# Attention with decay: a full reciprocal instead of a backward scan, the products moved to VectorE, four input buffers, one pass for transposing and gating

## The chip, the cores and the metric

The kernel runs on one core of one Trainium2 chip. The metric is the device time in microseconds, as the median of several runs. The engines are called here as the profile calls them: PE (TensorE), PEld (its weight loads), DVE (VectorE), ACT (ScalarE), POOL (GpSimd) and SP (SyncE, which issues the DMAs).

## The reference, cut to what matters

Three layers follow each other. The change touches the first alone.

```python
# q, k, v, alpha: (B, H, S, D) = (4, 8, 768, 48), fp32; alpha in 0.8 .. 1.0
state = np.zeros((B, H, D, D))
for t in range(S):
    state = alpha[:, :, t, :, None] * state + np.einsum('bhd,bhe->bhde', k[:, :, t], v[:, :, t])
    y[:, :, t] = np.einsum('bhd,bhde->bhe', q[:, :, t], state)
x = y.transpose(0, 2, 1, 3).reshape(B * S, H * D)          # (3072, 384)
logits = x @ w_gate                                        # (3072, 8)
# every token goes to one of 8 experts, best logits first, 384 tokens an expert;
# expert: relu(x @ w1[e]) @ w2[e];  after it: (silu(x @ w_gate2) * (x @ w_val)) @ w_out
```

## The kernel before, in words

**Units.** The attention cuts the 768 tokens of each batch into CH = 6 chunks of P = 128. A unit is one chunk of one batch; there are UNITS = 24, in the order chunk by chunk, and within a chunk batch by batch. `unit(i, j)` gives its number u = 4i + j, its batch b and its chunk c. The 8 heads of 48 channels lie as PAIRS = 4 pairs: the even head of a pair on partitions 0 to 47, the odd one on 64 to 111. The tokens lie along the free dimension, so q, k and alpha of a unit are each 128 x 512 values.

**The algebra.** Within a chunk, `decay` is the running product of alpha from the chunk's start (a scan along the tokens, L197, which starts each pair anew with the constant DECAY_UNIT). q is multiplied by it (`q_dec`, L261) and k by its inverse (`k_und`, L263). The inverse is not taken element by element: L204 takes the reciprocal of the last product of each pair alone (4 values a partition), and a second scan (L206) multiplies it by alpha backward from the chunk's end. For that the tokens of k, v and the scores' rows lie in reversed order, and a second, reversed copy of alpha is loaded. `qka_in` therefore holds 2052 words a row: q, k, alpha with a starting word for each pair, and alpha reversed.

**The rest of a unit.** PE multiplies `k_und` by `q_dec` (L359, `front`), which gives the scores, and turns `k_und` into rows of tokens (L366). DVE masks the scores (L215). PE's `outputs` adds two products in `ps_y_cols`: the state of the chunks before by `q_dec` (L376) and v by the masked scores (L383). For L376 ACT first writes the state of both heads of a pair into the two diagonal blocks of `state_pair` (L303), so that one product serves two heads. PE's `update` makes the chunk's share of the state (L393); DVE's `advance` adds it (L225) and scales the state with the chunk's decay (L229). ACT copies `ps_y_cols` to `y_cols` (L296). PE's `gate_and_turn` multiplies `y_cols` by the gate's weights (L401, 8 columns) and transposes it (L404). ACT copies the rows (L314, two copies) and the logits (L320), and SP stores the rows to `x_rows`.

**The order of work.** Each engine has its own stream of instructions, run in order and held by waits on semaphores. DVE's step j masks unit j+1 (`mask_scores`), makes the decays of unit j+3 (`decays`) and advances the state of unit j. PE's step j does `outputs(j)`, `update(j)`, `gate_and_turn(j-1)` and `front(j+2)`. POOL's `scale` follows the decays. SP loads unit u+2 when the keys of unit u have been scaled (`load_next`), since there are two `qka_in` buffers, then the next v of the batch, and then stores unit j. PE begins with WARMUPS = 22 matmuls on zeros.

**Beside the attention** run parts of the later layers: in each chunk two pieces of weights of 128 x 1152 are loaded and split into a high and a low part; the high parts are made by ACT (L1186), the low parts by DVE and POOL, one each (`split_gated_low`, L1190). The names `quick_...` from L631 on belong to the routing. It starts when the attention's block has ended on all engines, and its first instruction (L650) reads the finished `logits`. It and the expert layers stand behind the attention in time.

## Time and profile before

| | us |
|---|---|
| median of 3 runs | 970.67 |
| lowest and highest run | 968.34, 971.88 |
| the profiled execution, its own time | 969.62 |
| its span, from the first to the last instruction | 967.8 |
| first scan of the attention starts | 8.22 |
| first instruction of the routing starts | 204.66 |

All times inside the kernel come from the one profiled execution, counted from the start of its span. Its own time is 1.8 us longer than its span. The mean granted clock of PE over the span is 0.931 of full speed. Busy times of one engine do not add to those of another, as the engines run side by side; what a change is worth is read from the waits in its stretch.

### The profile page before, as it was taken

How to read it: one execution, taken by the hardware profiler on the slowest of the kernel's cores; microseconds unless marked ns; L12 is line 12 of the kernel's file. 1: busy time of each engine (PE TensorE's matmuls, PEld its weight loads, DVE VectorE, ACT ScalarE, POOL GpSimd, SP SyncE). 2: the span in 40 equal slices, each digit the busy share in tenths (PEclk: the TensorE clock that was granted, in tenths of full speed). 3: DMA queues.
4: the chain of work that ended last, by engine and by line, in shares of the span. 5: the costliest groups of instructions: out<-in, count | busy, mean ns of one | idle time of the engine just before them, and what ended most of it. 6: DMA issues, size and time to landing. Idle time of an engine off the chain costs nothing.

```text
span 967.8 us, 17835 instructions
## 1 busy us (share of the span) xinstructions
PE 880.0 (91%) x6586; PEld 836.5 (86%) x6586; DVE 547.3 (57%) x1077; ACT 299.2 (31%) x579; POOL 269.2 (28%) x195
## 2 busy tenths in 40 slices
PE   6798889841999999999999999999999999999991
PEld 3787878830999999999999999999999999999991
DVE  4988888846456446544644564465446445642330
ACT  1243343421323323333224233323332242333220
POOL 2444434411304140521224041305212240513001
PEclk7697798765899999999999999999999999999996
DMA  9787898604003101200220040013002200400000
GB/s 226 141 193 162 194 217 199 145 26 155 1 1 123 42 16 65 90 24 0 81 73 24 0 130 33 16 65 89 24 0 81 73 24 0 135 33 11 1 1 28
DMA packets 25250, 71.30 MB, mean 74 GB/s; under 512 B 4288, under 2 KB 10816, under 8 KB 22848
## 3 DMA queue, kind: packets, MB, share of 16 engines
q1 hardware_dynamic: 22144, 61.42, 24.9%
q0 software_dynamic: 3072, 9.44, 2.9%
q8 instruction: 20, 0.33, 0.2%
q14 instruction: 14, 0.11, 0.0%
HBM read 61.41 MB, written 9.44 MB: 73 GB/s over the span
## 4 chain that ended last, share of the span: by engine, by line
PE 72%; DVE 3%; issue 1%; DMA 1%; POOL 0%; ACT 0%; POOLq 0%; DVEq 0%; ACTq 0%
PE ps_up L1500 43%; PE ps_acc L1500 25%; PE ps_turn L784 2%; DVE quick_marks_space L709 1%; DMA x_tok<-x_rows,from_rows 1%; PE ps_turn L804 1%; PE ps_turn L1506 0%; PE ps_turn L789 0%; DVE quick_marks_space L761 0%; POOL out L1348 0%; PE ps_up L1506 0%; PE ps_acc L1506 0%; POOL x_tok L1320 0%; DVE quick_cut L708 0%; DVE quick_base L703 0%
## 5 line engine op out<-in xcount | busy, mean ns | idle before, releaser
L1326 POOL TENSOR_TENSOR w_low<-w_raw,w_high 128x768 fp32r<-128x768 f32 x60 | 134.3, 2244 | 295.9 <-ACT w_high L1390 295.4
L1500 PE MATMUL ps_up<-z_high,gated_high 128*128 128x384 f32 x576 | 198.0, 344 | 0.2 <-DVE z_low L1457 0.2
L1500 PE MATMUL ps_up<-z_high,gated_low 128*128 128x384 f32 x576 | 193.5, 336 | 0.0
L1500 PE MATMUL ps_up<-z_low,gated_high 128*128 128x384 f32 x576 | 193.3, 336 | 0.0
L1500 PEld LDWEIGHTS ps_up<-z_high,gated_high 128*128 128x128 f32 x576 | 108.2, 188 | 0.9 <-ACT z_high L1403 0.5
L1500 PEld LDWEIGHTS ps_up<-z_high,gated_low 128*128 128x128 f32 x576 | 108.3, 188 | 0.0
L1500 PEld LDWEIGHTS ps_up<-z_low,gated_high 128*128 128x128 f32 x576 | 108.1, 188 | 0.0
L1462 DVE TENSOR_TENSOR act_out<-ps_up,act_out 128x384 f32<-128x384 f32 x96 | 53.5, 558 | 94.6 <-ACT act_out L1406 91.9
L1409 ACT CAST u_high<-act_out 128x384 fp32r<-128x384 f32 x96 | 49.3, 514 | 160.3 <-DVE act_out L1466 160.3
L1500 PE MATMUL ps_acc<-gated_high,u_high 128*128 128x384 f32 x288 | 97.6, 339 | 0.3 <-DVE u_low L1469 0.3
L1500 PE MATMUL ps_acc<-gated_low,u_high 128*128 128x384 f32 x288 | 97.2, 337 | 0.0
L1500 PE MATMUL ps_acc<-gated_high,u_low 128*128 128x384 f32 x288 | 97.0, 337 | 0.0
L1406 ACT ACTIVATE act_out<-ps_up 128x384 f32<-128x384 f32 x96 | 47.3, 492 | 154.7 <-PE ps_up L1500 154.7
L1348 POOL DMA_INDIRECT out<-o_tok,to_rows x24 | 23.6, 985 | 224.7 <-ACT o_tok L1418 189.8
L1469 DVE TENSOR_TENSOR u_low<-act_out,u_high 128x384 fp32r<-128x384 f32 x96 | 53.6, 558 | 55.7 <-ACT u_high L1409 55.7
L1451 DVE SCALAR_TENSOR_TENSOR h_low<-ps_up,h_high 128x384 fp32r<-128x384 f32 x64 | 35.7, 557 | 83.3 <-ACT h_high L1386 81.2
L1466 DVE TENSOR_TENSOR act_out<-act_out,ps_up 128x384 f32<-128x384 f32 x96 | 53.3, 555 | 42.3 <-PE ps_up L1500 41.6
L1390 ACT CAST w_high<-w_raw 128x768 fp32r<-128x768 f32 x64 | 53.3, 833 | 63.4 <-PE ps_acc L1500 35.0
L1500 PE MATMUL ps_up<-x_high,w_high 128*128 128x384 f32 x192 | 68.8, 358 | 0.0
L1500 PE MATMUL ps_acc<-h_high,w_high 128*128 128x384 f32 x192 | 65.0, 338 | 0.0
L1500 PE MATMUL ps_up<-x_high,w_low 128*128 128x384 f32 x192 | 64.8, 338 | 0.0
L1500 PE MATMUL ps_up<-x_low,w_high 128*128 128x384 f32 x192 | 64.8, 337 | 0.0
(165 smaller groups left out, 1580.0 us busy)
## 6 DMA issues: line engine op xcount, KB each, us to landing
w_raw<-in_experts SPq DMA_DIRECT2D x64, 384.0 KB, 3.1
qka_in<-in_qka SPq DMA_DIRECT2D x44, 384.8 KB, 6.8
v_in<-in_v SPq DMA_DIRECT2D x24, 192.0 KB, 7.3
x_rows<-y_rows SPq DMA_DIRECT2D x24, 192.0 KB, 4.4
quick_marks_space<-in_gated SPq DMA_DIRECT2D x6, 576.0 KB, 5.8
gated_raw<-in_gated SPq DMA_DIRECT2D x6, 576.0 KB, 7.1
qka_in<-in_qka_first SPq DMA_DIRECT2D x4, 513.0 KB, 7.2
x_tok<-x_rows,from_rows POOLq DMA_INDIRECT x24, 3.2
```

The costliest lines, as they stand in the source:

```text
L709: dve.tensor_tensor(self.over_cut, self.best[:, :].unsqueeze(2).broadcast_to(tc), self.cut[:, :].unsqueeze(1).broadcast_to(tc), ALU.is_ge) ...
L784: mm = pe.matmul(self.ps_count[0:CUTS - 1, :], self.over_cut[:, t, :], self.choice[:, t, :], start=(t == 0), stop=(t == TILES - 1))
L1326: pool.tensor_tensor(w.low[:, m % RING, :], w.raw[:, m % RING, :], w.high[:, m % RING, :].bitcast(F32), ALU.subtract).then_inc(w_low_ready, 1)
L1348: pool.indirect_dma_start(out=out, out_offset=bass.IndirectOffsetOnAxis(ap=to_rows[:, t:t + 1], axis=0), in_=o_tok[:, t, :], in_offset=Non ...
L1390: act.copy(w.high[:, m % RING, :], w.raw[:, m % RING, :]).then_inc(w_high_ready, 1)
L1406: act.activation(act_out[:, j % 2, :], ps_up[j % 2][0][:, 0:CAP], ACT.Sigmoid).then_inc(sigm_ready, 1)
L1409: act.copy(u_high[:, j % 2, :], act_out[:, j % 2, :]).then_inc(u_high_ready, 1)
L1451: dve.scalar_tensor_tensor(out=h_low[:, m % 2, :], in0=ps_up[m % 2][0][:, 0:CAP], scalar=0.0, in1=h_high[:, m % 2, :].bitcast(F32), op0=AL ...
L1462: dve.tensor_tensor(act_out[:, j % 2, :], ps_up[j % 2][0][:, 0:CAP], act_out[:, j % 2, :], ALU.mult).then_inc(silu_ready, 1)
L1466: dve.tensor_tensor(act_out[:, j % 2, :], act_out[:, j % 2, :], ps_up[j % 2][1][:, 0:CAP], ALU.mult).then_inc(gated_ready, 1)
L1469: dve.tensor_tensor(u_low[:, j % 2, :], act_out[:, j % 2, :], u_high[:, j % 2, :].bitcast(F32), ALU.subtract).then_inc(u_low_ready, 1)
L1500: mm = pe.matmul(acc, lhs[a], rhs[b], start=(first and i == 0), stop=(last and i == 2))
```

## The change

- The backward scan, its starts (`undecay_starts`), the small reciprocal and the reversed copy of alpha go. The reciprocal is now taken of the whole `decay`, 128 x 512, straight into `k_und`, which is then multiplied by k in place. Tokens are no longer reversed.
- Both products (`q_dec`, `k_und`) are made by DVE inside `decays`. POOL has only its setting up and its share of the weight splits. `decays` now waits as well for the outputs of four units before (`y_cols_ready`) and for the turned keys of two units before (`kt_ready`), as the products on POOL did.
- `qka_in` has four buffers, one a batch, of 1600 words a row (1540 used). The first four units are loaded at the start with all 128 partitions; unit u+4 is loaded when the keys of u are scaled.
- `state_pair` and its copies go. `outputs` multiplies v first and then, head by head, `state` itself on 48 rows; in the first chunk, where the state is zero, that part is left out.
- Gate and transposition are one product: `turner` holds for each pair the identity (96 columns) and beside it the gate's 8 columns for that pair. The logits then come in four parts, one a pair, which ACT copies to `logit_parts` and DVE adds up after the last unit (8 reductions).
- The rows of y take one copy by ACT instead of two.
- `front` begins with FILLERS = 4 bf16 matmuls on zeros with 512 columns, into the scores' bank that is written next.
- The last chunk no longer turns keys or updates the state where nothing reads them.

```diff
 WARMUPS = 22
 SEG = P + 1
-QKA = 3 * PAIRS * P + PAIRS * SEG
-
-
-def attention(nc, qka_first, qka, v, w_gate, ident, causal, x_rows, logits, w, quick, consts):
+QKA = 1600
+ALPHA_AT = 2 * PAIRS * P
+HEADS2 = 2 * D
+TURN_N = HEADS2 + E
+FILLERS = 4
...
+            def load_first(b):
                 for g in range(2):
                     rows = slice(HALF * g, HALF * (g + 1))
-                    sp.dma_start(qka_in[r][rows, :], qka_first[r, rows, :]).then_inc(qka_loaded[r], 16)
+                    sp.dma_start(qka_in[b][rows, :], qka_first[b, rows, :]).then_inc(qka_loaded[b], 16)
...
             for b in range(B):
-                if b < 2:
-                    load_first(b)
+                load_first(b)
...
             def load_next(i, j):
                 u, b, c = unit(i, j)
                 sp.wait_ge(k_ready, u + 1)
-                load(u + 2, j % 2)
+                load(u + B, b)
...
-                if not (isinstance(i, int) and B * i + j + 5 >= UNITS):
+                if not (isinstance(i, int) and B * i + j + 3 + B >= UNITS):
...
-                if not (isinstance(u, int) and u < 2):
-
-                    dve.wait_ge(k_ready, u - 1)
-                dve.wait_ge(qka_loaded[j % 2], 32 * (2 * i + j // 2 + 1))
-                n = 2 * PAIRS * P
-                dve.tensor_tensor_scan(decay[b][:, :, :].rearrange("p a t -> p (a t)"), qka_in[b % 2][:, n:n + PAIRS * SEG],
+                    dve.wait_ge(y_cols_ready, u - 3)
+                dve.wait_ge(qka_loaded[b], 32 * (i + j // B + 1))
+                dve.tensor_tensor_scan(decay[b][:, :, :].rearrange("p a t -> p (a t)"),
+                                       qka_in[b][:, ALPHA_AT:ALPHA_AT + PAIRS * SEG],
                                        decay_starts[:, :, :].rearrange("p a t -> p (a t)"), 0.0,
                                        ALU.mult, ALU.add).then_inc(decay_ready, 1)
+
+                def part(n):
+                    return qka_in[b][:, n * PAIRS * P:(n + 1) * PAIRS * P].rearrange("p (a t) -> p a t", a=PAIRS)
+
+                if not (isinstance(u, int) and u < 2):
+
+                    dve.wait_ge(kt_ready, u - 1)
                 dve.wait_ge(decay_ready, u + 1)
-                if not (isinstance(u, int) and u == 0):
-
-                    dve.wait_ge(undecay_ready, u)
-                dve.reciprocal(undecay_starts[:, :, 0], decay[b][:, :, P]).then_inc(ends_ready, 1)
-                dve.wait_ge(ends_ready, u + 1)
-                dve.tensor_tensor_scan(undecay[b % 2][:, :, :].rearrange("p a t -> p (a t)"), qka_in[b % 2][:, n + PAIRS * SEG:],
-                                       undecay_starts[:, :, :].rearrange("p a t -> p (a t)"), 0.0,
-                                       ALU.mult, ALU.add).then_inc(undecay_ready, 1)
+                dve.reciprocal(k_und[b % 2][:], decay[b][:, :, 1:SEG]).then_inc(undecay_ready, 1)
+                dve.tensor_tensor(q_dec[b][:], part(0), decay[b][:, :, 1:SEG], ALU.mult).then_inc(q_ready, 1)
+                dve.wait_ge(undecay_ready, u + 1)
+                dve.tensor_tensor(k_und[b % 2][:], part(1), k_und[b % 2][:], ALU.mult).then_inc(k_ready, 1)
...
+            by_expert = [logit_parts[:, CH * b:CH * (b + 1), :, :].rearrange("p c a e -> p c e a") for b in range(B)]
+            dve.wait_ge(lg_copied, UNITS - B)
+            for b in range(B):
+                dve.tensor_reduce(logits[:, CH * b:CH * (b + 1) - 1, :], by_expert[b][:, 0:CH - 1], AX_X,
+                                  ALU.add).then_inc(lg_summed, 1)
+            for b in range(B):
+                dve.wait_ge(lg_copied, UNITS - B + b + 1)
+                dve.tensor_reduce(logits[:, CH * (b + 1) - 1, :], by_expert[b][:, CH - 1], AX_X,
+                                  ALU.add).then_inc(lg_summed, 1)
+            dve.wait_ge(lg_summed, 2 * B)
...
-            with pool.Fori(1, CH) as i:
-                for j in range(B):
-                    u, b, c = unit(i, j)
-
-                    pool.wait_ge(y_cols_ready, u - 3)
-                    pool.wait_ge(kt_ready, u - 1)
-                    scale(u, b)
-                    if j == 1:
-                        w.split_gated_low(pool, gated_raw, i - 1, 1)
-            w.split_gated_low(pool, gated_raw, CH - 1, 1)
+            with pool.Fori(0, CH) as i:
+                w.split_gated_low(pool, gated_raw, i, 1)
...
+                act.copy(y_rows[b % 2][:, :].rearrange("p (a n) -> p a n", a=PAIRS),
+                         y_turned_out[:, :, 0:HEADS2]).then_inc(y_copied, 1)
...
-                act.copy(logits[:, CH * b + c, :], ps_logits).then_inc(lg_copied, 1)
+                act.copy(logit_parts[:, CH * b + c, :, :], y_turned_out[:, :, HEADS2:TURN_N]).then_inc(lg_copied, 1)
...
-
-                    pe.wait_ge(k_tok_ready, u)
-                for a in range(PAIRS):
-                    tr = pe.transpose(ps_k[:, a * P:(a + 1) * P], k_und[j % 2][:, a, :], idt[:, :])
-                tr.then_inc(kt_ready, 1)
-
-            def outputs(i, j):
+                if keys:
+                    if j > 0 or started:
+
+                        pe.wait_ge(k_tok_ready, u)
+                    for a in range(PAIRS):
+                        tr = pe.transpose(ps_k[:, a * P:(a + 1) * P], k_und[j % 2][:, a, :], idt[:, :])
+                    tr.then_inc(kt_ready, 1)
+
+            def outputs(i, j, first_chunk=False):
 
                 u, b, c = unit(i, j)
-                if not (isinstance(u, int) and u < B):
-
-                    pe.wait_ge(state_paired, u - 3)
-                for a in range(PAIRS):
-                    pe.matmul(ps_y_cols[:, a * P:(a + 1) * P], state_pair[b][:, a, :], q_dec[b][:, a, :],
-                              start=(a == 0), stop=False)
+                if not first_chunk:
+
+                    pe.wait_ge(state_ready, u - 3)
                 pe.wait_ge(v_loaded[b], 16 * (c + 1))
                 pe.wait_ge(masked, u + 1)
                 for a in range(PAIRS):
                     for g in range(2):
                         h = 2 * a + g
-                        mm = pe.matmul(ps_y_cols[HALF * g:HALF * g + D, a * P:(a + 1) * P],
-                                       v_in[b][:, D * h:D * (h + 1)], scores[j % 2][:, h, :], start=False, stop=(a == PAIRS - 1))
+                        mm = pe.matmul(ps_y_cols[HALF * g:HALF * g + D, a * P:(a + 1) * P], v_in[b][:, D * h:D * (h + 1)],
+                                       scores[j % 2][:, h, :], start=(a == 0), stop=(first_chunk and a == PAIRS - 1))
+                if not first_chunk:
+                    for a in range(PAIRS):
+                        for g in range(2):
+                            rows = slice(HALF * g, HALF * g + D)
+                            mm = pe.matmul(ps_y_cols[rows, a * P:(a + 1) * P], state[b][rows, a, :],
...
 
             def gate_and_turn(i, j):
-                u, b, c = unit(i, j)
                 for a in range(PAIRS):
-                    pe.matmul(ps_logits, y_cols[j % 2][:, a * P:(a + 1) * P], wg[:, a, :],
-                              start=(a == 0), stop=(a == PAIRS - 1))
-                for a in range(PAIRS):
-                    tr = pe.transpose(ps_y_rows[:, a * (HALF + D):a * (HALF + D) + P],
-                                      y_cols[j % 2][:, a * P:(a + 1) * P], idt[:, :])
-                tr.then_inc(y_turned, 1)
-
-            def step(i, j, first=False, ahead=True):
...
+                mm.then_inc(y_turned, 1)
+
+            def step(i, j, first=False, first_chunk=False, ahead=True, keys=True, updated=True):
                 u, b, c = unit(i, j)
                 if not first:
 
                     pe.wait_ge(y_cols_copied, u)
-                outputs(i, j)
-                if not first:
-
-                    pe.wait_ge(state_ready, u)
-                update(i, j)
+                outputs(i, j, first_chunk)
+                if updated:
+                    if not first:
+
+                        pe.wait_ge(state_ready, u)
+                    update(i, j)
                 if not first:
...
             pe.wait_ge(consts_in, 16 * 2)
             front(0, 0, started=False)
             front(0, 1, started=False)
-            pe.wait_ge(zeroed, 2 * B + 1)
             for j in range(B):
-                step(0, j, first=(j == 0))
+                step(0, j, first=(j == 0), first_chunk=True)
```

## Rows read from the trace of the kernel before

**Rows 1.** The page: busy us (share of the span) and instructions of each engine.

```profile
PE 880.0 (91%) x6586; PEld 836.5 (86%) x6586; DVE 547.3 (57%) x1077; ACT 299.2 (31%) x579; POOL 269.2 (28%) x195
```

**Rows 2.** Windows: busy us (instructions) per engine, clock, DMA share, GB/s, the body.

```profile
8.00:185.00 177.00, 146.92 (x1534) 132.09 (x1536) 149.56 (x162) 61.26 (x153) 79.84 (x55) 0.80 0.85 186
```

**Rows 3.** Waits in the body: us in total, times, longest us.

```profile
DVE decay L197 <- DMA qka_in<-in_qka: 22.1, 10, 6.8
...
DVE decay L197 <- DMA qka_in<-in_qka_first: 5.2, 2, 2.9
```

**Rows 4.** Groups of DVE, 0 to 205 us: busy us, mean ns, idle before.

```profile
L206 DVE TENSOR_TENSOR_SCAN undecay<-qka_in,undecay_starts 128x512 f32<-128x512 f32 x24 | 55.7, 2321 | 0.8
L215 DVE TENSOR_TENSOR scores<-ps_scores,mask 128x512 f32<-128x512 f32 x48 | 30.6, 676 | 0.1
L197 DVE TENSOR_TENSOR_SCAN decay<-qka_in,decay_starts 128x516 f32<-128x516 f32 x24 | 29.5, 1230 | 27.3 <-DMA qka_in<-in_qka 22.1 <-DMA qka_in<-in_qka_first 5.2
L229 DVE SCALAR_TENSOR_TENSOR state<-state,decay 128x192 f32<-128x192 f32 x24 | 27.7, 1154 | 0.8
L1190 DVE TENSOR_TENSOR gated_low<-quick_marks_space,gated_high 128x1152 f32 (+1 forms) x6 | 8.1, 1348 | 1.7 <-ACT gated_high L1186 1.7
L225 DVE TENSOR_TENSOR state<-ps_state,state 128x192 f32<-128x192 f32 x24 | 7.9, 330 | 2.1 <-PE ps_state L393 2.1
L204 DVE RECIPROCAL undecay_starts<-decay 128x4 f32<-128x4 f32 x24 | 4.3, 181 | 1.3
```

**Rows 5.** Timeline of DVE and POOL near 107, 189 and 194 us: start, us.

```profile
106.86 1.19 POOL L261 TENSOR_TENSOR q_dec<-qka_in,decay 128x512 f32<-128x512 f32 x1 [5.28 <-DVE decay L197]
107.03 2.10 DVE L206 TENSOR_TENSOR_SCAN undecay<-qka_in,undecay_starts 128x512 f32<-128x512 f32 x1
...
188.73 0.36 DVE L229 SCALAR_TENSOR_TENSOR state<-state,decay 128x192 f32<-128x192 f32 x1
...
194.34 2.69 DVE L229 SCALAR_TENSOR_TENSOR state<-state,decay 128x192 f32<-128x192 f32 x1
```

**Rows 6.** Groups of DVE by form, whole span: small and medium instructions.

```profile
L1469 DVE TENSOR_TENSOR u_low<-act_out,u_high 128x384 fp32r<-128x384 f32 x96 | 53.6, 558 | 55.7 <-ACT u_high L1409 55.7
...
L742 DVE TENSOR_TENSOR quick_rank<-quick_rank,quick_mine 128x24 f32<-128x24 f32 x8 | 1.5, 182 | 0.3
...
L692 DVE COPY quick_base<-quick_low 128x1 f32<-128x1 f32 x8 | 1.2, 154 | 0.3
```

**Rows 7.** Windows of the body, columns as in rows 2.

```profile
110.00:120.00 10.00, 9.23 (x64) 8.36 (x66) 9.90 (x11) 4.46 (x11) 6.98 (x4) 0.52 0.69 154
...
120.00:140.00 20.00, 17.80 (x228) 15.89 (x224) 16.10 (x19) 7.46 (x20) 6.25 (x7) 0.98 0.98 214
...
160.00:180.00 20.00, 16.67 (x161) 14.81 (x160) 17.54 (x18) 6.96 (x16) 9.72 (x7) 0.80 1.00 204
```

**Rows 8.** Timeline of PE: the bf16 warm-up's last weight loads, one unit near 125 us.

```profile
4.55 2.75 PEld L429 LDWEIGHTS ps_y_cols<-scores 128*128 128x128 bf16 x13 [0.27 <-issue]
...
122.91 1.16 PE L359 MATMUL ps_scores<-q_dec,k_und 48*128 48x128 f32 x16
...
126.94 1.06 PE L401 MATMUL ps_y_rows<-wg,y_cols 128*128 128x8 f32 x8
127.86 0.64 PE L404 MATMUL ps_y_rows<-quick_idt,y_cols 128*128 128x128 f32 x4
128.42 1.16 PE L359 MATMUL ps_scores<-q_dec,k_und 48*128 48x128 f32 x16
```

**Rows 9.** Timeline of DVE: the first scan, and the end of the attention.

```profile
8.22 1.23 DVE L197 TENSOR_TENSOR_SCAN decay<-qka_in,decay_starts 128x516 f32<-128x516 f32 x1 [2.90 <-DMA qka_in<-in_qka_first]
...
182.72 2.10 DVE L206 TENSOR_TENSOR_SCAN undecay<-qka_in,undecay_starts 128x512 f32<-128x512 f32 x1
...
192.05 1.28 DVE L215 TENSOR_TENSOR scores<-ps_scores,mask 128x512 f32<-128x512 f32 x2
...
204.66 0.35 DVE L650 TENSOR_REDUCE quick_ends<-logits 128x1 f32<-128x192 f32 x1 [6.10 <-PEq L39]
```

More of the change, by code:

```diff
@@ L30, with attention @@
 SEG = P + 1
-QKA = 3 * PAIRS * P + PAIRS * SEG
-def attention(nc, qka_first, qka, v, w_gate, ident, causal, x_rows, logits, w, quick, consts):
+QKA = 1600
[3 more added lines that the diff above has]
+FILLERS = 4
+def attention(nc, qka_first, qka, v, turn_gate, ident, causal, x_rows, logits, w, quick, consts):
     with ExitStack() as ctx:
@@ L47, in sem @@
             return ctx.enter_context(nc.semaphore(name))
-        qka_in = [sb(f"qka_in{r}", [P, QKA]) for r in range(2)]
+        qka_in = [sb(f"qka_in{b}", [P, QKA]) for b in range(B)]
         v_in = [sb(f"v_in{b}", [P, DM]) for b in range(B)]
@@ L53, in attention @@
         decay_starts = sb("decay_starts", [P, PAIRS, SEG])
-        undecay_starts = sb("undecay_starts", [P, PAIRS, P])
-        undecay = [sb(f"undecay{r}", [P, PAIRS, P]) for r in range(2)]
         q_dec = [sb(f"q_dec{b}", [P, PAIRS, P]) for b in range(B)]
@@ L58, in attention @@
         state = [sb(f"state{b}", [P, PAIRS, D]) for b in range(B)]
-        state_pair = [sb(f"state_pair{b}", [P, PAIRS, P]) for b in range(B)]
         y_rows = [sb(f"y_rows{r}", [P, DM]) for r in range(2)]
@@ L80, in attention @@
         mask_in = sem("mask_in")
-        qka_loaded = [sem(f"qka_loaded{r}") for r in range(2)]
+        qka_loaded = [sem(f"qka_loaded{b}") for b in range(B)]
         v_loaded = [sem(f"v_loaded{b}") for b in range(B)]
@@ L296, in y_cols_copy @@
                 act.copy(y_cols[j % 2][:], ps_y_cols[:, :]).then_inc(y_cols_copied, 1)
-            def state_pairs(i, j):
-                u, b, c = unit(i, j)
-                act.wait_ge(state_ready, u + 1)
-                for g in range(2):
-                    rows = slice(HALF * g, HALF * g + D)
-                    both = act.copy(state_pair[b][rows, :, rows], state[b][rows, :, :])
-                both.then_inc(state_paired, 1)
             def y_copy(i, j):
@@ L327, in step @@
                     lg_copy(i, j - 1)
-                state_pairs(i, j)
                 if ahead:
@@ L347, in _, with front @@
         def _(pe):
-            def front(i, j, started=True):
+            def front(i, j, started=True, keys=True):
                 u, b, c = unit(i, j)
@@ L353, in front @@
                     pe.wait_ge(masked, u - 1)
+                    for n in range(FILLERS):
+                        pe.matmul(ps_scores[j % 2][0][:, :], warm[:, 0:P], warm[:], start=True, stop=True)
                 pe.wait_ge(q_ready, u + 1)
@@ L439, in _ @@
             for j in range(B):
-                step(CH - 1, j, ahead=(j < 2))
+                step(CH - 1, j, ahead=(j < 2), keys=False, updated=(j == 0))
             pe.wait_ge(y_cols_copied, UNITS)
@@ L453, in lay_out_attention, with lay_out_turner @@
     seg[..., 1:] = aa
-    back = np.zeros((CH, B, 2, D, PAIRS, P), np.float32)
-    back[..., 1:] = aa[..., :0:-1]
-    flat = lambda a: a.reshape(CH, B, 2, D, -1)
-    qka = np.concatenate([flat(qq), flat(kk[..., ::-1]), flat(seg), flat(back)], axis=-1).reshape(UNITS, 2, D, QKA)
-    first = np.zeros((2, 2, HALF, QKA), np.float32)
-    pad_seg, pad_back = np.ones((PAIRS, SEG), np.float32), np.ones((PAIRS, P), np.float32)
-    pad_seg[:, 0] = pad_back[:, 0] = 0.0
-    first[..., 2 * PAIRS * P:] = np.concatenate([pad_seg.reshape(-1), pad_back.reshape(-1)])
-    first[:, :, :D] = qka[:2]
-    vv = np.ascontiguousarray(v.reshape(B, H, CH, P, D)[:, :, :, ::-1].transpose(2, 0, 3, 1, 4)).reshape(UNITS, P, DM)
-    return first.reshape(2, P, QKA), qka[2:], vv
-def lay_out_gate(w):
-    pad = np.zeros((2, HALF, PAIRS, E), np.float32)
-    pad[:, :D] = w.reshape(PAIRS, 2, D, E).transpose(1, 2, 0, 3)
-    return pad.reshape(P, PAIRS, E)
+    qka = np.zeros((CH, B, 2, D, QKA), np.float32)
+    for at, a in ((0, qq), (PAIRS * P, kk), (ALPHA_AT, seg)):
+        a = a.reshape(CH, B, 2, D, -1)
+        qka[..., at:at + a.shape[-1]] = a
+    qka = qka.reshape(UNITS, 2, D, QKA)
+    first = np.zeros((B, 2, HALF, QKA), np.float32)
+    pad_seg = np.ones((PAIRS, SEG), np.float32)
+    pad_seg[:, 0] = 0.0
+    first[..., ALPHA_AT:ALPHA_AT + PAIRS * SEG] = pad_seg.reshape(-1)
+    first[:, :, :D] = qka[:B]
+    vv = np.ascontiguousarray(v.reshape(B, H, CH, P, D).transpose(2, 0, 3, 1, 4)).reshape(UNITS, P, DM)
+    return first.reshape(B, P, QKA), qka[B:], vv
+def lay_out_turner(w):
+    turner = np.zeros((2, HALF, PAIRS, TURN_N), np.float32)
+    for a in range(PAIRS):
+        for g in range(2):
+            h = 2 * a + g
+            turner[g, :D, a, D * g:D * (g + 1)] = np.eye(D)
+            turner[g, :D, a, HEADS2:] = w[D * h:D * (h + 1)]
+    return turner.reshape(P, PAIRS, TURN_N)
 BIG = 1e38
@@ L1593, in _, with build @@
                 expert(E - 1, last=True)
-def build(nc, qka_first, qka, v, w_gate, ident, causal, experts, gated, consts, out):
+def build(nc, qka_first, qka, v, turn_gate, ident, causal, experts, gated, consts, out):
     x_rows = nc.dram_tensor("x_rows", [N, DM], F32, kind="Internal").ap()
```

66 lines of the change are left out of this document (23 added, 43 removed).

## The prediction

> **What bounds the kernel now.** I began with the busy shares of the page [rows 1]: PE 91% of the span. That average belongs to the two layers behind the attention, which the change leaves alone, so I cut the trace in two. Between 8 and 185 us, the body of the attention, PE is busy 146.9 of 177 us at 0.80 of its clock, VectorE (DVE) 149.6, the DMA engines 0.85 [rows 2]. No engine is full, so I asked what ended the waits. DVE waits 22.1 us for `qka_in` loads and 5.2 us for the first ones [rows 3]. 149.6 busy and 27.3 waiting make 176.9 of 177.0 us: in this stretch DVE never waits for anything but loads. The 24 units (a batch's chunk of 128 tokens each) take 7.4 us apiece there: 6.2 of DVE's work, 1.1 of waiting for loads.
>
> Then the groups of DVE [rows 4]: per unit a scan (L197, 1.23 us), a reciprocal of 4 values (L204, 0.18), a second scan (L206, 2.32), two mask products (L215, 0.68 each), an addition (L225, 0.33) and the state's scaling (L229, 1.15). Two of these are dearer than their size. The second scan has 512 elements, the first 516, and takes twice as long. The timeline shows why [rows 5]: GpSimd's product L261 starts at 106.86 and lasts 1.19 us, and L206 beside it takes 2.10. L229 took 0.36 us with GpSimd idle, but 2.69 at 194.34, where GpSimd's weight split (L1190) ran.
>
> **The change, part by part.** The same sum for the kernel after, over the stretch from the first scan to unit 23's last scaled product:
>
> Removed from DVE: second scans 55.7, small reciprocals 4.3 us [rows 4]. GpSimd loses both products, so what they held up goes: L229 falls towards 0.36 [rows 5].
>
> Added to DVE per unit: two products of 128x512 with both inputs in SBUF, and one reciprocal of 128x512. Products: 384 elements take 558 ns [rows 6], 1152 take 1348 [rows 4], so 1.03 ns an element, and 512 take 0.69 us: 48 x 0.69 = 33.1.
>
> The reciprocal R decides the case, and its large form is nowhere in the trace. The small one takes 181 ns for 4 elements [rows 4]. Beside it [rows 6]: a copy of 1 element, 154 ns; a product of 24 elements, 182 ns. An ordinary instruction of 4 should take 154 to 161, so 20 to 27 ns too many lie on 4 elements. Three readings: fixed part 157 (from the product of 24: 182 - 24 x 1.03), 5.9 ns an element, R = 3.2 us; fixed part 153 (from the copy), 7.0 ns an element, R = 3.74; the first element inside the copy's 154 and three more of 9.0 ns, R = 4.75. The extra could also be one fixed delay: then R = 0.69 + 0.03 = 0.72. I take 3.9: near the reading from the copy (like this one, it has one input), moved up as the third reading is open. For the range I keep 3.2 to 4.75, and 0.72 as a rival.
>
> The Trainium skill ("VectorE: DVE Perf Modes", Walkthrough: the 8-slice pipeline in each mode) says that the reciprocal is an iterated divide with a repeat count of 8. Taken as eight steps an element at that page's 0.96 GHz, R would be an estimated 4.4 us and the time about 1002; the 181 ns lie just under what that gives, and no run here shows the large form yet.
>
> The sum: first scans 29.5; products 33.1; masks of 22 units at 1.28 a pair [rows 9] 28.2; 20 additions 6.6; 20 scalings at 0.36 7.2; 5 weight splits at 1.35 6.7; together 111.3 + 24R. The same adding up for before (with 55.7, 4.3 and 23.9 for L229) gives 154.9, where the trace has 149.6 busy, since neighbours overlap by hundredths; I take the same 5 off: 106 + 24R. GpSimd's five splits remain and can each hold a DVE instruction by up to 2.3 us; half the time DVE is in the reciprocal, with one input. I take 1 us each, 5 in all (0 to 11). So 111 + 24R; with 3.9, 204.6 us, or 8.5 a unit against 7.4.
>
> Start: the first scan begins at 8.22 [rows 9] behind 1.05 MB; the rows are now 1600 instead of 2052 words, so 0.82 MB; at 0.21 to 0.25 MB/us 0.9 to 1.1 us earlier, I take 7.3. Units 2 and 3 are now issued at once, not behind the first scaled keys, so DVE's longest wait for loads (6.8 us) [rows 3] goes.
>
> Tail: before, 19.85 us pass from the end of the last second scan (184.81) to the routing's first instruction (204.66) [rows 9], with PE behind. After: state advance 0.7, mask 1.28, weight split 1.36, mask 1.28; then both output products 2.1, copy 0.6, turn 1.1, copy 0.5, and an estimated 2.5 for the store's landing and the block's end. That is 11.2, I take 11.3.
>
> Routing starts at 7.3 + 111 + 24R + 11.3 = 129.6 + 24R = 223.2 us against 204.66: 18.5 later. It decides at R = 3.1 us. After it nothing changes. The profiled execution took 969.6 us (span 967.8), so 988.1; the median of the runs is 1.1 higher, so about **989**.
>
> At nothing, and what covers it:
> - Loads. A unit needs 0.61 (was 0.79) MB of `qka_in`, 0.2 of `v_in`, 0.3 of gated weights and 0.2 stored, 1.3 MB. At 204 to 214 GB/s in the full windows [rows 7] that is 6.2 us, under 8.5. Unit u+4's load waits for unit u's k, a wait that is three units early. Without this cover a unit costs the difference.
> - PE. At full clock one unit takes 5.51 us (122.91 to 128.42) [rows 8]. The state products stay at what they take, in smaller pieces; gate 1.06 and transposes 0.64 become one pass of about 1.06; four zero matmuls add 0.85 (13 of them in 2.75 us) [rows 8]: 5.7. Under 8.5, and update(j) has a whole DVE step before it is late.
> - ACT loses two state copies and a y copy a unit and was 35% busy (61.3 us) [rows 2]. The last chunk's keys, updates and first chunk's state products go, all beside DVE, except three advances that lay in the tail.
> - DVE's new wait for `kt_ready` is on the transposes of two units before; behind it are the reciprocal, both products, the advance and next mask, and PE waits for those. PE does it one DVE step earlier, so it is met.
> - The eight sums of the logits, 2 us, run beside PE's last outputs and the last store.
>
> **Rivals.**
> 1. The reciprocal runs at about one element a step, R = 0.72. For it: nothing shows the large form. Against: 181 ns is above every comparable small row. Then DVE needs 111 + 17 = 128 us and the loads bind: about 32.6 MB instead of 36.3, at 209 GB/s (the middle of [rows 7]) 156 us, with first latency and a tail not read from memory about 168 to 172 instead of 204.66: **936**. It decides the other way as soon as R is below 3.1. The Trainium skill's "Vector Engine (DVE) Microarchitecture Reference" (3.2 Anatomy of a single slice) says that the divide chain spans all eight slices; if each slice took one step of it, an element could leave every step, which is this rival. It and the reading above can't both give the rate; the trace favours the slow one. Chance 0.18.
> 2. PE falls to half clock in the idle 2.8 us that each unit now leaves it. Twice 5.7 is 11.5 us a unit, 3 more than DVE. For it: the clock did halve, with a mean of 0.80 [rows 2] and 0.52 from 110 to 120 us [rows 7]. Against: PE was 9.2 of 10 us busy in that stretch and was at 0.98 in the next [rows 7], so it comes back when it is full; each stretch begins with a whole step of slack; and the zero matmuls fill 0.85 us. Four such stretches, each 3 to 4 us beyond the slack, add 14: **1003**. Chance 0.12.
> 3. R at the bottom of its reading, 3.1 to 3.3, with fewer collisions: the loss per unit is what the loads' waits were, and the time is **970 to 975**. Chance 0.10.
>
> Forecast (DVE bound by a reciprocal of 3.3 to 4.75 us): chance 0.60. Its own range: R = 3.3 gives 975, R = 4.75 gives 1009.
>
> **How the numbers follow.** Half a per cent, 4.9 us, is about what a measurement of this kernel can tell from no change. Slower: the forecast 0.60, rival 2 0.12, a quarter of rival 3, so 0.74. Same: 0.08. Faster: 0.18. Range: 968 to 1010 holds forecast, most of rivals 2 and 3, and leaves out rival 1 and the tips, near 2 in 10. Where the likeliest case fails, the time is outside on the low side.
>
> **What would show it.** The reciprocal's mean (3.2 to 4.75 us; under 3.1 overturns the sign); the product rows at 0.69; L229's mean near 0.4; no wait of DVE for `qka_in` behind the first; DVE over 0.95 busy in the body, 8.5 us from scan to scan; PE idle 2 to 3 us a unit, waiting for DVE's state; DMA share near 0.65; the routing starting at about 223 us. A clock of 0.5 with PE full and DVE waiting for `ps_state` or scores would be rival 2. DMA share at 1 with a beat near 6.2 us would be rival 1.

## The result, and the profile after

The change made the kernel slower: 981.0 us median (979.3 to 982.3), against 970.7 before, a ratio of 1.0108 with a 95% interval of 1.0083 to 1.0133. Run again with five rounds, it gave 979.4 against 969.5, ratio 1.0102 (1.0087 to 1.0117). The profiled execution took 981.15 us, its span is 977.6. The routing's first instruction moved from 204.66 to 214.99 us, 10.3 later; what follows it took 762.6 us (before 763.1), and the time outside the span grew from 1.8 to 3.5 us.

The window of the body in the changed kernel, from the first scan to the last scaled keys (columns as in [rows 2]):

```profile
8.00:201.00 193.00, 146.26 (x1666) 113.59 (x1688) 190.46 (x187) 46.92 (x93) 17.62 (x7) 0.89 0.67 156
```

VectorE (DVE) is busy 190.5 of 193 us, where it was busy 149.6 of 177 [rows 2]; the DMA share went from 0.85 to 0.67. The waits from 8 to 200 us:

```profile
PE ps_state L371 <- DVE state L228: 31.0, 17, 4.2
...
DVE decay L192 <- DMA qka_in<-in_qka_first: 5.1, 1, 5.1
```

The 22.1 us of waiting for `qka_in` [rows 3] are gone altogether; only the first load is waited for (5.1 us, before the first scan). PE now waits 31 us for the state, that is for DVE. The groups of DVE, against [rows 4]:

```profile
L204 DVE RECIPROCAL k_und<-decay 128x512 f32<-128x512 f32 x24 | 80.5, 3353 | 1.0
L214 DVE TENSOR_TENSOR scores<-ps_scores,mask 128x512 f32<-128x512 f32 x48 | 30.8, 682 | 0.5 <-issue 0.2
L192 DVE TENSOR_TENSOR_SCAN decay<-qka_in,decay_starts 128x516 f32<-128x516 f32 x24 | 30.6, 1274 | 5.1 <-DMA qka_in<-in_qka_first 5.1
L207 DVE TENSOR_TENSOR k_und<-qka_in,k_und 128x512 f32<-128x512 f32 x24 | 16.4, 682 | 0.0
L228 DVE SCALAR_TENSOR_TENSOR state<-state,decay 128x192 f32<-128x192 f32 x21 | 15.6, 744 | 0.7
L205 DVE TENSOR_TENSOR q_dec<-qka_in,decay 128x512 f32<-128x512 f32 x24 | 15.1, 630 | 0.0
L1169 DVE TENSOR_TENSOR gated_low<-quick_marks_space,gated_high 128x1152 f32 (+1 forms) x6 | 8.1, 1350 | 1.1 <-ACT gated_high L1165 0.8 <-issue 0.3
L224 DVE TENSOR_TENSOR state<-ps_state,state 128x192 f32<-128x192 f32 x21 | 7.4, 351 | 0.0
```

The full reciprocal takes 3353 ns, 24 times 80.5 us. It stands in the place of the backward scan (55.7) and the small reciprocal (4.3). The products add 31.5 us. The state's scaling fell from 27.7 to 15.6 us, not to 7.5: its rows in the timeline are 0.36 us long except in four units (2.38), where GpSimd (POOL) splits weights beside it and holds it up, as here (DVE and POOL near 115 us):

```profile
114.48 3.12 POOL L1169 TENSOR_TENSOR gated_low<-gated_raw,gated_high 128x1152 f32 x1 [30.49 <-ACT gated_high L1165]
...
115.43 2.38 DVE L228 SCALAR_TENSOR_TENSOR state<-state,decay 128x192 f32<-128x192 f32 x1
...
117.74 1.35 DVE L1169 TENSOR_TENSOR gated_low<-quick_marks_space,gated_high 128x1152 f32 x1
```

L228, 0.36 us by itself, ends at 117.81, 0.2 us behind the POOL instruction's end at 117.60. The start, against [rows 9]:

```profile
7.71 1.23 DVE L192 TENSOR_TENSOR_SCAN decay<-qka_in,decay_starts 128x516 f32<-128x516 f32 x1 [5.10 <-DMA qka_in<-in_qka_first]
8.98 3.35 DVE L204 RECIPROCAL k_und<-decay 128x512 f32<-128x512 f32 x1
...
19.06 1.23 DVE L192 TENSOR_TENSOR_SCAN decay<-qka_in,decay_starts 128x516 f32<-128x516 f32 x1
```

Unit 2's scan starts at 19.06 with no wait; before, it stood until 24.42. The end of the attention (DVE and PE):

```profile
200.01 0.68 DVE L207 TENSOR_TENSOR k_und<-qka_in,k_und 128x512 f32<-128x512 f32 x1
...
203.87 1.08 PE L355 MATMUL ps_y_cols<-scores,v_in 128*48 128x128 f32 x16 [1.25 <-ACT y_cols L280]
...
204.64 1.28 DVE L214 TENSOR_TENSOR scores<-ps_scores,mask 128x512 f32<-128x512 f32 x2
...
205.88 1.14 PE L378 MATMUL ps_y_rows<-turner,y_cols 128*128 128x104 f32 x8
...
206.95 1.08 PE L355 MATMUL ps_y_cols<-scores,v_in 128*48 128x128 f32 x16
...
207.96 1.08 PE L361 MATMUL ps_y_cols<-q_dec,state 48*48 48x128 f32 x16
...
210.91 1.11 PE L378 MATMUL ps_y_rows<-turner,y_cols 128*128 128x104 f32 x8 [0.80 <-ACT logit_parts L293]
...
214.99 0.35 DVE L629 TENSOR_REDUCE quick_ends<-logits 128x1 f32<-128x192 f32 x1 [2.07 <-PEq L43]
```

From the end of the last scaled keys (200.69) to the routing are 14.3 us. PE's rows show why. The outputs of unit 22 start only at 203.87, 1.25 us held by ACT's copy of `y_cols`; the turn of unit 21 (205.88) follows. So the outputs of unit 23 (206.95, and 207.96 for its state part) start 1.0 us after DVE's last mask has ended (204.64 + 1.28). The last turn (210.91) waits 0.8 us more, for ACT's copy of unit 22's logits.

### The profile page after: what moved, and what is told of

Same layout as the page of the kernel before. It is cut to its first block, busy times and chain, and to the rows that moved or that the text cites. A ratio compares the mean times of both kernels' runs of the same rounds, so it can differ in the third digit from the quotient of the medians.

```text
span 977.6 us, 17767 instructions
## 1 busy us (share of the span) xinstructions
PE 873.2 (89%) x6628; PEld 811.5 (83%) x6650; DVE 581.3 (59%) x1098; ACT 280.9 (29%) x505; POOL 206.4 (21%) x147
## 3 DMA queue, kind: packets, MB, share of 16 engines
q1 hardware_dynamic: 22208, 57.75, 22.1%
## 4 chain that ended last, share of the span: by engine, by line
PE 72%; DVE 2%; issue 1%; DMA 1%; POOL 0%; ACT 0%; POOLq 0%; ACTq 0%
PE ps_up L1479 43%; PE ps_acc L1479 26%; PE ps_turn L763 2%; DMA x_tok<-x_rows,from_rows 1%; PE ps_turn L783 1%; PE ps_turn L1485 0%; DVE quick_marks_space L688 0%; PE ps_turn L768 0%; DVE quick_marks_space L740 0%; POOL out L1327 0%; PE ps_up L1485 0%; PE ps_acc L1485 0%; POOL x_tok L1299 0%; DVE quick_cut L687 0%; DVE quick_base L682 0%
## 5 line engine op out<-in xcount | busy, mean ns | idle before, releaser
L1479 PE MATMUL ps_acc<-gated_low,u_high 128*128 128x384 f32 x288 | 97.2, 337 | 0.0
L1448 DVE TENSOR_TENSOR u_low<-act_out,u_high 128x384 fp32r<-128x384 f32 x96 | 53.6, 559 | 55.7 <-ACT u_high L1388 55.7
L204 DVE RECIPROCAL k_und<-decay 128x512 f32<-128x512 f32 x24 | 80.5, 3353 | 1.0
```

The costliest lines, as they stand in the source:

```text
L204: dve.reciprocal(k_und[b % 2][:], decay[b][:, :, 1:SEG]).then_inc(undecay_ready, 1)
L1448: dve.tensor_tensor(u_low[:, j % 2, :], act_out[:, j % 2, :], u_high[:, j % 2, :].bitcast(F32), ALU.subtract).then_inc(u_low_ready, 1)
L1479: mm = pe.matmul(acc, lhs[a], rhs[b], start=(first and i == 0), stop=(last and i == 2))
```

## The experiments

Every time is given with the ratio to the kernel before, from the same rounds; the changed kernel stands at 1.0108 and 1.0102.

**1. The reciprocal replaced by a multiplication.**

```diff
-dve.reciprocal(k_und[b % 2][:], decay[b][:, :, 1:SEG]).then_inc(undecay_ready, 1)
+dve.tensor_scalar(k_und[b % 2][:], decay[b][:, :, 1:SEG], 2.0 ** -80, None, ALU.mult).then_inc(undecay_ready, 1)
```

> The changed kernel, with the full reciprocal replaced by a multiplication of the running product by 2^-80 (128 x 512, one input). It leaves out the inverse, so the attention it computes is another one. Theory (the reciprocal of 3.35 us on VectorE is the beat): an instruction of about 0.4 us in its place frees 24 x 2.9 = 70 us of VectorE, more than can be won, because the loads (32.6 MB at about 209 GB/s, 156 us) or PE (5.8 us a unit at full clock) bind next; the routing starts at 165 to 175 us instead of 215 and the time is 931 to 941 us. Rival (the slowdown sits in the zero matmuls, the half clock or the moved products, and the reciprocal only fills time in which VectorE would wait): the time stays within 5 us of 981.

The whole time, 1871 us, says nothing here: the kernel leaves out the inverse, so its logits are other ones. The quick routing did not settle them, and the exact routing and both layers once more ran behind it. The attention's own stretch can be read. The routing starts at 166.35 us:

```profile
166.35 0.35 DVE L629 TENSOR_REDUCE quick_ends<-logits 128x1 f32<-128x192 f32 x1 [2.08 <-PEq L43]
```

That is 48.6 us earlier than with the reciprocal, so the rival falls. What binds next (window 40 to 140 us of this kernel, and DVE's largest wait in it):

```profile
40.00:140.00 100.00, 98.24 (x1260) 77.01 (x1275) 91.53 (x136) 36.30 (x72) 11.03 (x5) 1.00 0.88 211
...
DVE scores L214 <- PE ps_scores L333: 6.7, 7, 1.5
```

PE is busy 98.2 of 100 us at a clock of 1.00, and DVE waits for its scores and for no load; DVE is at 91.5 and the DMA engines at 0.88. I had named loads or PE; it is PE.

**2. Both products back on GpSimd.**

DVE then waits for the product of q of four units before, and GpSimd for the outputs of four units before, as in the kernel before.

```diff
-dve.wait_ge(y_cols_ready, u - 3)
+dve.wait_ge(q_ready, u - 3)
...
-dve.tensor_tensor(q_dec[b][:], part(0), decay[b][:, :, 1:SEG], ALU.mult).then_inc(q_ready, 1)
-dve.wait_ge(undecay_ready, u + 1)
-dve.tensor_tensor(k_und[b % 2][:], part(1), k_und[b % 2][:], ALU.mult).then_inc(k_ready, 1)
...
+pool.wait_ge(decay_ready, u + 1)
+pool.tensor_tensor(q_dec[b][:], part(0), decay[b][:, :, 1:SEG], ALU.mult).then_inc(q_ready, 1)
+pool.wait_ge(undecay_ready, u + 1)
+pool.tensor_tensor(k_und[b % 2][:], part(1), k_und[b % 2][:], ALU.mult).then_inc(k_ready, 1)
...
```

> The changed kernel with both products back on GpSimd, the reciprocal kept. Theory (VectorE is the beat, and it and GpSimd hold each other when both read two inputs from SBUF): VectorE loses 0.63 + 0.68 us a unit; the product of q runs on GpSimd under the reciprocal, which has one input, and costs nothing; the product of k (about 1.28 us on GpSimd) holds the state's scaling for about 0.9 us. Net -0.4 us a unit, -10 us: about 971 us. Rival A (moving the products was free because VectorE was not the bound): 981 within 3. Rival B (no holding at all): -1.3 x 24 = -31 us, 950.

974.2 us, ratio 1.0045 (1.0028 to 1.0062), some 6 us faster than the changed kernel; the routing starts at 207.1. The timeline, DVE first and then POOL:

```profile
105.19 3.35 DVE L204 RECIPROCAL k_und<-decay 128x512 f32<-128x512 f32 x1
108.46 0.29 DVE L221 TENSOR_TENSOR state<-ps_state,state 128x192 f32<-128x192 f32 x1
108.79 1.32 DVE L225 SCALAR_TENSOR_TENSOR state<-state,decay 128x192 f32<-128x192 f32 x1
...
105.24 1.18 POOL L264 TENSOR_TENSOR q_dec<-qka_in,decay 128x512 f32<-128x512 f32 x1 [2.85 <-DVE decay L192]
108.62 1.27 POOL L266 TENSOR_TENSOR k_und<-qka_in,k_und 128x512 f32<-128x512 f32 x1 [2.20 <-DVE k_und L204]
```

The product of q (105.24) starts with the reciprocal. It takes 1.17 to 1.19 us in all 24 units, and the reciprocal stays at 3.35. The product of k starts at 108.62 and ends at 109.89, and the state's scaling beside it lasts 1.32 instead of 0.36 us. Both parts of the theory stand. The gain came out 3 to 4 us short of the 10 forecast. In this kernel DVE's own weight split grew from a mean of 1.35 to 2.56 us, held as well (6 x 1.2 = 7 us). That this is what is missing is argued and not shown, since other rows moved too.

**3. No zero matmuls.**

```diff
-FILLERS = 4
+FILLERS = 0
```

> The changed kernel without the four zero matmuls. Theory (PE has about 2 us of slack a unit behind VectorE): no change, 981 within 2 us, whatever the clock does. Rival (the zero matmuls keep the clock up, and without them PE, at 9.7 us a unit at half clock, becomes the beat in part): 5 to 15 us slower, with VectorE waiting for scores or ps_state. Rival (the zero matmuls themselves delay the path): 2 to 5 us faster, in the tail and the start.

978.6 us, ratio 1.0084 (1.0051 to 1.0118): no difference that these intervals tell. The window 40 to 200 us:

```profile
40.00:200.00 160.00, 125.85 (x1432) 105.74 (x1432) 158.14 (x157) 41.53 (x84) 13.81 (x5) 0.83 0.61 143
```

The granted clock fell to 0.83, from 0.93 in the same window of the changed kernel, and DVE stayed at 158.1 of 160 us. The zero matmuls do hold the clock up (the mean over the whole span is 0.925 to 0.929 without them, 0.939 to 0.949 with them), and it is worth nothing that can be measured while DVE's work sets the pace.

**4. The backward scan in the changed kernel.** All else stays, four buffers too. The scan reads alpha backward out of the copy that is there anyway, so nothing more is loaded, and its starts lie in a free column of `decay_starts`; what they add to the next unit's forward scan is, by my estimate, far under fp32's rounding. The product of q now stands before the scan, and `k_und` is one column a pair wider.

```diff
-dve.reciprocal(k_und[b % 2][:], decay[b][:, :, 1:SEG]).then_inc(undecay_ready, 1)
+dve.reciprocal(decay_starts[:, :, P], decay[b][:, :, P]).then_inc(ends_ready, 1)
 dve.tensor_tensor(q_dec[b][:], part(0), decay[b][:, :, 1:SEG], ALU.mult).then_inc(q_ready, 1)
+dve.wait_ge(ends_ready, u + 1)
+dve.tensor_tensor_scan(k_und[b % 2][:, :, :].rearrange("p a t -> p (a t)")[:, ::-1],
+                       qka_in[b][:, ALPHA_AT + 1:ALPHA_AT + 1 + PAIRS * SEG][:, ::-1],
+                       decay_starts[:, :, :].rearrange("p a t -> p (a t)")[:, ::-1], 0.0,
+                       ALU.mult, ALU.add).then_inc(undecay_ready, 1)
...
```

> The changed kernel with the backward scan of the kernel before in place of the full reciprocal, everything else as changed. alpha is read backward from the copy that is loaded anyway, so no further bytes are loaded. Theory: VectorE's unit loses 3.35 us and gains 0.18 + 1.22, -1.95 us a unit, -47 us, so VectorE needs about 146 us from its first scan; then the loads (156 us) bind, and the routing starts at 168 to 178 us: 934 to 946 us. Rival 1 (the other parts of the change are what made it slow): the scan variant stays above 965. Rival 2 (PE at a lowered clock binds once VectorE is faster): 946 to 960, with VectorE waiting for ps_state or scores.

937.2 us, ratio 0.966 (0.9626 to 0.9693): faster than both kernels. Groups of DVE, the body's window, and the routing's start:

```profile
L193 DVE TENSOR_TENSOR_SCAN decay<-qka_in,decay_starts 128x516 f32<-128x516 f32 x24 | 37.0, 1542 | 6.5 <-DMA qka_in<-in_qka_first 6.2 <-DMA qka_in<-in_qka 0.3
...
L208 DVE TENSOR_TENSOR_SCAN k_und<-qka_in,decay_starts 128x516 f32<-128x516 f32 x24 | 29.5, 1228 | 0.0
...
L205 DVE RECIPROCAL decay_starts<-decay 128x4 f32<-128x4 f32 x24 | 4.3, 181 | 1.0
```

```profile
8.00:155.00 147.00, 131.95 (x1641) 103.57 (x1660) 141.79 (x209) 46.90 (x93) 14.86 (x7) 0.95 0.87 199
```

```profile
171.12 0.35 DVE L635 TENSOR_REDUCE quick_ends<-logits 128x1 f32<-128x192 f32 x1 [2.07 <-PEq L43]
```

The backward scan takes 1.23 us with GpSimd out of its way (2.32 before, [rows 4]), and the routing starts 43.9 us earlier than in the changed kernel, where the sum had 47. DVE's work still sets the beat of the units (6.1 us each), 141.8 of 147 us, with PE at 132.0 close behind at a clock of 0.95. So the full reciprocal, against a backward scan in its place, costs 44 us, and the rest of the change, taken together, is worth 33.5 us of the attention (204.66 to 171.12). How the rest divides among its parts is only partly told, by experiments 8 to 10.

**5. GpSimd's split started under the reciprocal.**

```diff
-with pool.Fori(0, CH) as i:
+with pool.Fori(0, CH - 1) as i:
+    pool.wait_ge(w.gated_high_ready[1], i + 1)
+    pool.wait_ge(decay_ready, B * i + 7)
     w.split_gated_low(pool, gated_raw, i, 1)
+w.split_gated_low(pool, gated_raw, CH - 1, 1)
```

> The changed kernel; GpSimd's weight split of the first five chunks waits until a unit's forward scan is done, so that it starts together with that unit's reciprocal (3.35 us, one input from SBUF) instead of wherever ScalarE happens to finish. Theory (GpSimd and VectorE hold each other only where VectorE reads two inputs from SBUF): the split runs in its 2.6 us beneath the reciprocal, the state's scaling falls from a mean of 0.74 to 0.36 us and the scan from 1.27 to 1.22: 9 us less, about 972. Rival (the holding is by any VectorE instruction): the reciprocal grows to some 5 us in five units, or the split to over 3 us, and the time stays at 981 within 2.

971.2 us, ratio 1.0019 (1.0006 to 1.0032), 8 to 10 us faster than the changed kernel, by the start of one instruction in each of five chunks. The timeline:

```profile
115.40 3.35 DVE L204 RECIPROCAL k_und<-decay 128x512 f32<-128x512 f32 x1
115.58 2.63 POOL L1172 TENSOR_TENSOR gated_low<-gated_raw,gated_high 128x1152 f32 x1 [29.04 <-DVE decay L192]
...
118.67 0.63 DVE L205 TENSOR_TENSOR q_dec<-qka_in,decay 128x512 f32<-128x512 f32 x1
```

The split takes 2.63 us (3.12 in the changed kernel at 114.48, 2.64 at 205.54) and the reciprocal beside it 3.35, as everywhere else. L228's mean is 0.36 and the forward scan's 1.22. So in these runs the reciprocal, with one input from SBUF, is not held by GpSimd's split, and the scaling and the scan, with two, are. The Trainium skill ("SBUF — State Buffer", Who interferes with whom) states the same rule for VectorE instructions with one and with two SBUF inputs. These rows agree with it.

**6. Later weight splits in the last chunk.**

ACT's splits move two units on; DVE's goes behind its first four sums of the logits.

```diff
-if j == 1:
-    w.split_gated_low(dve, gated_raw, CH - 1, 0)
...
+w.split_gated_low(dve, gated_raw, CH - 1, 0)
...
-step(CH - 1, j, ahead=False, split_after={0: 0, 1: 1})
+step(CH - 1, j, ahead=False, split_after={2: 0, 3: 1})
```

> The changed kernel; in the last chunk ScalarE and VectorE make their weight splits two units later, so that ScalarE does not stand before the copy of y_cols of unit 21 until the last gated weights have landed (5.9 us of idleness there). Theory (the tail of 14.3 us between the last scaled keys and the routing, where I had worked out 11.3, holds 3 us of this wait): 2 to 3 us faster, about 978.5. Rival (the stores and the block's end set the tail): no change.

978.5 us, ratio 1.0093 (1.0074 to 1.0111), not to be told from the changed kernel (the forecast's 978.5 was counted from 981.0; the changed kernel again gave 979.4). In the trace the stretch that was to shrink did not: from the end of the last scaled keys to the routing are still 14.6 us.

```profile
198.79 0.68 DVE L207 TENSOR_TENSOR k_und<-qka_in,k_und 128x512 f32<-128x512 f32 x1
...
206.01 1.08 PE L354 MATMUL ps_y_cols<-scores,v_in 128*48 128x128 f32 x16
...
207.02 1.08 PE L360 MATMUL ps_y_cols<-q_dec,state 48*48 48x128 f32 x16
...
209.97 1.11 PE L377 MATMUL ps_y_rows<-turner,y_cols 128*128 128x104 f32 x8 [0.80 <-ACT logit_parts L292]
...
214.05 0.35 DVE L628 TENSOR_REDUCE quick_ends<-logits 128x1 f32<-128x192 f32 x1 [2.07 <-PEq L43]
```

ACT no longer waits for the weights, and PE's own queue takes the time nevertheless: the outputs of unit 22 (from 202.92), the turn of 21, the outputs of 23 (206.01 and 207.02) and the turn of 22 follow each other without a gap, and the last turn (209.97) waits 0.80 us for a copy. PE also came to it later: unit 23's scores start 2.4 us behind the last scaled keys, 0.8 in the changed kernel. From those scores to the routing are 12.2 us instead of 13.5, so ACT's wait was worth about 1.3 us there, and the later start took it up. The profiled execution was the slowest of the six (980.2; the quickest took 977.3), so the times leave a gain of 1 to 2 us open, and no row shows one.

**7. Two buffers instead of four.**

```diff
-qka_in = [sb(f"qka_in{b}", [P, QKA]) for b in range(B)]
+qka_in = [sb(f"qka_in{r}", [P, QKA]) for r in range(2)]
...
-load(u + B, b)
+load(u + 2, j % 2)
...
```

> The changed kernel with two input buffers instead of four, the load of unit u+2 waiting for the scaled keys of unit u as before the change; rows stay 1600 words. Theory (with VectorE's beat at 7.5 to 8 us the loads, 6.2 us a unit, fit with either number of buffers once running; the buffers matter at the start, where unit 2's load is issued 5 us later than its scan could begin): 4 to 8 us slower than the changed kernel, 985 to 989, the wait sitting at units 2 and 3. Rival (the four buffers are what took away all of the 27 us of waiting for loads): 15 to 27 us slower, with waits of about 1 us in most units.

983.2 us, ratio 1.0141 (1.0117 to 1.0164): 3 to 4 us slower than the changed kernel, a little under the 4 to 8 forecast. The only wait that came back is unit 2's, 3.2 us:

```profile
21.49 1.23 DVE L195 TENSOR_TENSOR_SCAN decay<-qka_in,decay_starts 128x516 f32<-128x516 f32 x1 [3.21 <-DMA qka_in<-in_qka_first]
```

**8. Experiment 4 without the zero matmuls.** Same edit as in experiment 3.

> The backward scan in the changed kernel (the fourth experiment), without the four zero matmuls. There PE is 19.1 of 20 us busy and VectorE 19.6. Theory (VectorE stays the beat, and PE without 0.85 us of zeros has more slack, but its clock may fall): 937 within 3 us as long as the clock stays up. Rival (the zero matmuls hold the clock, and at half clock PE needs 9.7 us a unit against VectorE's 5.7): 5 to 20 us slower, with VectorE waiting for scores or ps_state.

939.7 us, ratio 0.9692 (0.9672 to 0.9712), against 0.966 (0.9626 to 0.9693) with them: slower by 2 to 3 us if at all. In the profiled execution, the slowest of the five (941.8), the routing starts at 176.56 instead of 171.12. The intervals overlap, so a small use of the zero matmuls is likely and not shown.

**9. Experiment 4 with the products on GpSimd.** The edit of experiment 2 on the kernel of experiment 4.

> The backward scan in the changed kernel (the fourth experiment, 937), with both products moved back to GpSimd as in the kernel before. Theory (the products belong on VectorE only because they and the scans hold each other): VectorE loses 0.67 + 0.69 us a unit of products and gains 0.9 in the second scan, held by the product of q, and 0.9 in the state's scaling, held by the product of k: +0.4 us a unit, 10 us slower, about 947, with a mean of 2.1 us for the backward scan and 1.2 for the scaling. Rival (the products' place makes no difference, the loads or PE bind at 937): within 3 us of 937. Rival (GpSimd takes load off VectorE): 5 to 20 us faster.

946.3 us, ratio 0.9764 (0.9746 to 0.9781). Both rows are as worked out:

```profile
L209 DVE TENSOR_TENSOR_SCAN k_und<-qka_in,decay_starts 128x516 f32<-128x516 f32 x24 | 52.1, 2171 | 0.8
...
L233 DVE SCALAR_TENSOR_TENSOR state<-state,decay 128x192 f32<-128x192 f32 x21 | 23.6, 1123 | 0.7
```

So moving the products to DVE is worth 9 to 10 us beside a scan, and cost about 6 beside the reciprocal (experiment 2).

**10. Experiment 4 with two buffers.** The edit of experiment 7 on the kernel of experiment 4.

> The backward scan in the changed kernel (the fourth experiment, 937), with two input buffers instead of four. Theory (with VectorE's beat at 6.2 us a load of two DMAs that takes 5 to 7 us to land after the keys of two units before is just late again): VectorE waits for qka_in in many units, 0.3 to 1 us each, and at the start; 8 to 20 us slower, 945 to 957. Rival (as in the seventh experiment, two buffers are enough once running): 2 to 4 us slower, the wait at the start only.

944.8 us, ratio 0.974 (0.9721 to 0.9759), 7.6 us slower than with four, just under the range of the theory and above that of the rival. The place speaks for the rival (waits of DVE from 8 to 170 us):

```profile
DVE decay L196 <- DMA qka_in<-in_qka_first: 10.6, 3, 5.0
...
DVE decay L196 <- DMA qka_in<-in_qka: 1.0, 3, 0.4
```

The waits sit in the first three units; in the steady part there is 1.0 us in all. The profiled execution was the quickest of the five (941.1), so some of the 7.6 us is not in this trace. Between 40 and 140 us DVE is busy 97.2 of 100 us here, so two buffers are enough even at this short beat. Of the 33.5 us of experiment 4, the four buffers, the place of the products (experiment 9) and the zero matmuls (experiment 8) account for some 20, each taken away by itself; the shorter rows of `qka_in` and the other parts were not tried singly.

**11. The changed kernel again.**

> The changed kernel itself once more, on the same chip and in the same rounds as the kernel before, to narrow its difference: 10 to 11 us slower by all theories; the routing starts at 215 us within 1.

Its result stands at the top; the routing starts at 213.7 us.

## Why the prediction was right

The prediction's bound, path and sign were right, and the size was within its range: 989 forecast, 981.0 measured. Its sum was 7.3 + 111 + 24R + 11.3. The trace has 7.71, then 193.0 with 24R = 80.5, so 112.5 for the 111, then 14.3: 215.0. The miss of 8 us is smaller than its largest error, by luck: the reciprocal was taken 13 us too dear, and the start, the body and the tail together 5 us too cheap, with 1.7 more outside the span. With the measured R the forecast's own sum has the routing 5.4 us later than before; the other half of the 10.3 came from terms that it had too small.

- **What bounds the kernel: right.** DVE's work and its waits for loads filled the body before; the waits went and the work took their place. Experiments 1 and 4 replaced the one instruction (4 also puts the product of q before the scan) and got the time back.
- **The reciprocal: the kind right, the size 0.55 us too high.** It was 3.9 in the sum and is 3.353 us: 13 us of the sum, the largest error in it. With 181 ns for 4 elements [rows 4], 508 more elements cost 3172 ns, 6.24 ns each, over a fixed part of 156. Of the three readings the first was the nearest, the one that took the fixed part from a product of 24 elements (5.9 ns, 157 ns, R = 3.2). I had moved upward from the copy's reading, for which no row spoke. The Trainium skill ("VectorE: DVE Perf Modes", Walkthrough: the 8-slice pipeline in each mode) names a repeat count of 8. At that page's 0.96 GHz, 6.24 ns are an estimated 6.0 cycles, so eight steps an element, as I had read it, is not what was measured; the measurement decides.
- **The products: right.** 0.69 forecast, 0.63 and 0.68 measured, partly overlapping.
- **Collisions with GpSimd's split: the mechanism right, the size too small.** 5 us in the sum; L228 alone lost 8 us and the scan 1. They met the state's scaling and not, as I had argued, the reciprocal half of the time: ACT's high part releases the split at the same point of each round (80.88, 114.48, 148.10 and 181.70 us, 33.6 apart). Experiment 5 moved it and got 8 to 10 us back. The 111 came out at 112.5 all the same, since the products were 1.6 us cheaper and neighbours overlapped by some 9 us where 5 had been taken off; that is an offset and not foresight.
- **The tail: 3 us too short.** The sum ran DVE's steps without a gap, then unit 23's outputs and turn without a wait. In the trace DVE waits 0.8 us for ACT's high part before its last split, PE is still busy with unit 22's outputs and unit 21's turn for 1.0 us after the last mask, and the last turn starts 1.2 us after the copy of `y_cols` has ended. A first guess put the 3 us on ACT's wait for the last weights; experiment 6 took that wait away, and the tail stayed.
- **Nothing after the routing: right; nothing outside the span: wrong** by 1.7 us. It goes with the zero matmuls, which are all that experiment 3 takes away: there it is 1.8 us again.
- **Loads covered: right.** No wait behind the first. But the four buffers are not what did it: with two (experiment 7) only unit 2 waits. Nor is the longer beat needed: in experiment 10, with two buffers and the short beat back, the loads behind the first ones are waited for by 1.0 us, against 22.1 before. That leaves the shorter rows and the keys scaled by DVE, which no run tells apart.
- **Rival 1 (the cheap reciprocal, 936): fell by the row of 3353 ns.** Experiment 1 shows that with a cheap instruction the routing would have started at 166.4 us, a little before its 168 to 172, though with PE as the next bound and not the loads.
- **Rival 2 (PE at half clock): did not happen.** The clock did fall in places (0.53 from 20 to 30 us, 0.70 from 80 to 90), but DVE stayed busy there, 9.8 and 9.9 of 10 us; its mean was 0.89 in the body, and without the zero matmuls it fell further without cost (experiment 3).
- **Rival 3 (R from 3.1 to 3.3, 970 to 975): came near.** R was 3.35, and the tail and the collisions put the time above it.

## What to carry to other kernels

Replacing an instruction with a shorter program by one whose size the trace does not show is decided by its time per element: take that from the smallest form that is there, with the fixed part of another small instruction of the same engine taken off. When one engine's work sets the pace, shorten the one instruction and keep the rest of the change: here the rest was worth 3.4%, and the reciprocal took all of it and 1% more. Where two engines hold each other, look at what the other engine's instruction lands on; putting GpSimd's split beneath an instruction with a single SBUF input was worth 0.8 to 0.9%.

## What the runs showed of the hardware that I had not expected

- A reciprocal on VectorE costs 6.24 ns an element (181 ns for 128x4, 3353 for 128x512), the forward scan 2.1 (1.23 us for 516 less the same fixed part), a product 1.03.
- A scan whose three operands all run backward takes the same 1.23 us (experiment 4).
- The time outside the span was 1.7 to 1.9 us in the profiled executions of the kernel before and of the two kernels without zero matmuls in the attention, 2.0 in experiment 1, and 2.6 to 3.9 in all the others. Experiments 3 and 8 take away the zero matmuls alone, and with them go 1 to 2 us of it; experiment 1 has them, though, and is at 2.0. Nothing in the trace shows where the time lies, and no run tells why.
